# A delta-rule recurrence: the state update from B as two rounds of quarter-row matmuls, and two loads at another place

## The reference, cut to what matters

```python
batch, n_heads, seq, head_dim = (4, 8, 768, 40)

def _attn_ref(r, k, v, w, a, b):
    for t in range(S):
        y[:, :, t] = np.einsum('bhd,bhde->bhe', rt, state)
        Sa = np.einsum('bhde,bhe->bhd', state, at)
        state_decay = state * wt[:, :, None, :] - np.einsum('bhd,bhe->bhde', Sa, bt)
        state = state_decay + np.einsum('bhd,bhe->bhde', vt, kt)

def reference(**kwargs):
    attn_out = _attn_ref(**attn_kwargs)                        # 32 heads, a 40x40 state each
    x = attn_out.transpose(0, 2, 1, 3).reshape(B * S, H * D)   # 3072 tokens of 320
    x = _moe_ref(x=x, **moe_kwargs)     # gate: x @ w_gate + log1p(exp(x @ w_noise)) * noise, the best 2 of 8
    return _moe2_ref(x=x, **moe2_kwargs)                       # dense 320 -> 2048 -> 320
```

## Time and profile before

| what | value |
|---|---|
| median of 3 runs | 1462.92 us (1461.02 to 1466.77) |
| profiled execution | 1462.92 us, span 1461.1 us |
| stage_a, stage_re up to its first expert matmul, the rest | 0 to 541 us, 541 to 588 us, 588 to 1461 us |
| mean granted TensorE clock over the span | 0.926 of full speed |

### The profile page before, as it was taken

How to read it: one execution, slowest core, us unless ns; L and a number is a source line. 1 busy time by engine, 2 the same in 40 slices (tenths; PEclk the granted TensorE clock), 3 DMA queues, 4 the chain that set the end, 5 groups by cost and what they waited for, 6 DMA issues and landing times. The chain is left out here.

```text
span 1461.1 us, 37835 instructions
## 1 busy us (share of the span) xinstructions
PE 1270.4 (87%) x15278; PEld 1159.1 (79%) x15278; DVE 947.4 (65%) x1619; ACT 666.1 (46%) x1453; POOL 304.3 (21%) x262
## 2 busy tenths in 40 slices
PE   4458789778887966999999999999939999999998
PEld 3447577666776755999999999999938888888987
DVE  8978685795938017788788788887825535455343
ACT  3325444444543330567666676776603333333332
POOL 1116262542623221111111111111042012020000
PEclk9998888888988875999999999999969999999999
DMA  6563535536243312877877778778521011010000
GB/s 228 143 161 99 144 119 139 169 111 167 92 113 114 91 25 71 259 239 226 263 229 248 254 210 265 246 226 254 167 77 42 23 33 54 1 54 18 0 19 18
DMA packets 158832, 197.61 MB, mean 135 GB/s; under 512 B 62869, under 2 KB 117373, under 8 KB 158717
## 3 DMA queue, kind: packets, MB, share of 16 engines
q1 hardware_dynamic: 136724, 148.12, 33.5%
q10 hardware_dynamic: 16713, 29.77, 6.5%
q0 software_dynamic: 5280, 18.03, 4.3%
HBM read 171.57 MB, written 24.31 MB: 134 GB/s over the span
## 5 line engine op out<-in xcount | busy, mean ns | idle before, releaser
L350 DVE TENSOR_TENSOR prod<-Tl,Lt 128x1 f32<-128x1 f32 (+30 forms) x186 | 151.9, 817 | 51.4 <-DMA Lt<-lscr 45.3
L1297 DVE TENSOR_TENSOR gf<-psM,low 128x512 f32<-128x512 f32 x96 | 66.3, 691 | 181.1 <-ACT low L1335 169.4
L1335 ACT ACTIVATE low<-psM 128x512 f32<-128x512 f32 x96 | 57.5, 599 | 244.3 <-PE psM L1393 223.5
L1001 PE MATMUL psE<-w2h,hh 128*128 128x320 f32 x496 | 155.7, 314 | 0.0
L1003 PE MATMUL psE<-w2h,hl 128*128 128x320 f32 x496 | 153.3, 309 | 0.0
L1002 PE MATMUL psE<-w2l,hh 128*128 128x320 f32 x496 | 153.2, 309 | 0.0
L1089 POOL DMA_INDIRECT xs<-xrow,src x62 | 60.9, 982 | 410.2 <-PE psE L970 370.8
L986 PE MATMUL psE<-xh,w1h 128*128 128x256 f32 x496 | 141.1, 285 | 1.9 <-DVE xh L833 1.9
L987 PE MATMUL psE<-xl,w1h 128*128 128x256 f32 x496 | 141.0, 284 | 0.0
L988 PE MATMUL psE<-xh,w1l 128*128 128x256 f32 x496 | 140.9, 284 | 0.0
L833 DVE TENSOR_TENSOR w2l<-w2t,w2h 128x320 fp32r<-128x320 f32 x248 | 122.0, 492 | 16.3 <-ACT w2h L828 16.3
(11 more groups left out here) (185 smaller groups left out, 3154.8 us busy)
## 6 DMA issues: line engine op xcount, KB each, us to landing
w2t<-in_w_dram SPq DMA_DIRECT2D x31, 1280.0 KB, 6.8
w1t<-in_w_dram SPq DMA_DIRECT2D x31, 1024.0 KB, 8.9
w1t<-in_w_dram SPq DMA_DIRECT2D x62, 256.0 KB, 9.4
Vd<-in_vG_dram ACTq DMA_DIRECT2D x44, 320.0 KB, 4.8
ysort<-ys SPq DMA_DIRECT2D x31, 320.0 KB, 5.0
RV<-in_rvE_dram ACTq DMA_DIRECT2D x44, 208.0 KB
P<-in_wR_dram SPq DMA_DIRECT2D x24, 209.6 KB
U<-in_wE_dram SPq DMA_DIRECT2D x24, 209.6 KB
```

The lines of the kernel that those rows point to most:

```text
L350: mark(nc.vector.tensor_tensor(prod[:, 0:t, 0:t], Tl[:, 0:t, CH - t:CH], Lt[:, t:t + 1, CH - t:CH].to_broadcast([128, t, t]), ALU.mult))
L1001: mm(o, hh[:, f, sl], w2h[:, f, :], start=(f == 0), stop=False)
```

## The change

Four edits.

1. Pn loses its zeroed copies: it is [128, 4, 2, 40] instead of [128, 4, 2, 2, 40]. ACT still makes two copies a chunk, each of 160 elements a partition instead of 320, with the constant scale -1. half_m is gone. `turn_P` writes its four transposes 104 columns apart instead of 128.
2. `grow_B` contracts over one quarter (32 partitions) at a time, 40 columns, so it has 32 matmul calls a chunk instead of 16. They stand in two rounds: quarters 0 and 2, and then, behind a wait on o_S for the end of the first round, quarters 1 and 3. A call of float32 is two weight loads and two matmuls in the trace.
3. noise and triu are loaded by ACT's queue at the start of `stage_a`, triu in the place of half_m, noise last; nz and triu are allocated for the whole program. The DMAs on SP and the waits on r_nz and r_tu are gone; ACT waits for noise at the end of `stage_a`.
4. The constants array loses its last two columns.

```diff
-        half_m = sb("half_m", [128, 2])
-        Pn = sb("Pn", [128, 4, 2, 2, D])
+        Pn = sb("Pn", [128, 4, 2, D])
@@ ScalarE, start of stage_a
             act.dma_start(ident[:, :], cst[:, 0:128]).then_inc(q["l_c"], 16)
-            act.dma_start(half_m[:, :], cst[:, 480:482]).then_inc(q["l_c"], 16)
+            act.dma_start(triu[:, :], cst[:, 128:256]).then_inc(q["l_c"], 16)
...
             act.dma_start(wx[:, :, :], wgh[:, :, :]).then_inc(q["l_c"], 16)
+            act.dma_start(st["nz"][:, :, :], noise.rearrange("(i p) e -> p i e", p=128)).then_inc(q["l_nz"], 16)
@@ ScalarE, each chunk
-                for z in range(2):
-                    copy(Pn[:, :, :, z, :].rearrange("p g x d -> p (g x) d"), ps[:, 6, :].rearrange("p (g m) -> p g m", m=64)[:, :, 0:D],
-                         "a_Pn" if z else None, scale=half_m[:, z:z + 1])
+                for x in range(2):
+                    copy(Pn[:, :, x, :], ps[:, 6, 0:4 * EP].rearrange("p (g m) -> p g m", g=4)[:, :, 64 * x:64 * x + D],
+                         "a_Pn" if x else None, scale=-1.0)
@@ ScalarE, end of stage_a
+            act.wait_ge(q["l_nz"], 16)
@@ TensorE
-                    m = turn(ps[:, 6, 128 * i:128 * i + EP], PTs[:, i, :], unit)
+                    m = turn(ps[:, 6, EP * i:EP * i + EP], PTs[:, i, :], unit)
-            def grow_B(k):
+            def grow_B(k, f):
                 s, c = slot(k)
                 for b in range(NB):
                     for p in range(2):
-                        for i in range(2):
-                            two = slice(64 * i, 64 * i + 64)
-                            m = mm(ps[E_[p], i, 0:2 * NB * D].rearrange("p (z m) -> p z m", z=2)[:, :, D * b:D * b + D],
-                                   Bk[two, (4 * s + c) % RT, b, p, :], Pn[two, 2 * (b // 2) + p, b % 2, :, :].rearrange("p z d -> p (z d)"),
+                        for h in (f, f + 2):
+                            o = (h % 2) * NB * D + D * b
+                            m = mm(ps[E_[p], h // 2, o:o + D], Bk[Z_[h], (4 * s + c) % RT, b, p, :], Pn[Z_[h], 2 * (b // 2) + p, b % 2, :],
                                    start=False, stop=True, skip_group_check=True)
-                m.then_inc(q["p_S"], 1)
+                m.then_inc(q["p_S" if f else "o_S"], 1)
...
                     pe.wait_ge(q["a_Pn"], k + 1)
-                    pe.wait_ge(q["o_S"], k + 1)
-                    grow_B(k)
+                    pe.wait_ge(q["o_S"], 2 * k + 1)
+                    grow_B(k, 0)
+                if k < NK:
+                    pe.wait_ge(q["o_S"], 2 * k + 2)
+                    grow_B(k, 1)
@@ stage_re: SyncE, TensorE, VectorE
-            sp.dma_start(nz, noise.rearrange("(i p) e -> p i e", p=128)).then_inc(q["r_nz"], 16)
-            sp.dma_start(triu[:, :], cst[:, 128:256]).then_inc(q["r_tu"], 16)
-            pe.wait_ge(q["r_tu"], 16)
-            dve.wait_ge(q["r_nz"], 16)
```

More of the change, by code:

```diff
@@ L43, with stage_a @@
 KE = [(0, 128), (128, 128), (256, 64)]
-def stage_a(nc, st, wE, wR, aE, bE, kE, rvE, vG, cst, wgh, lscr, tscr, xrow):
+def stage_a(nc, st, wE, wR, aE, bE, kE, rvE, vG, cst, wgh, noise, lscr, tscr, xrow):
     ctx = ExitStack()
@@ L55, in stage_a @@
         ps = ctx.enter_context(nc.psum_tensor("psA", [128, 8, 512], F32))
-        LG, ident = st["LG"], st["ident"]
+        LG, ident, triu = st["LG"], st["ident"], st["triu"]
         pos_m = sb("pos_m", [128, CH])
-        half_m = sb("half_m", [128, 2])
         two_m = sb("two_m", [128, 2, CH])
@@ L88, in stage_a @@
         xo = sb("xo", [128, 2, DM])
-        names = ("l_c l_p l_p0 l_p1 l_p2 l_p3 l_u0 l_u1 l_u2 l_a0 l_a1 l_a2 l_b0 l_b1 l_k0 l_k1 l_r0 l_r1 l_r2 l_g0 l_g1 "
+        names = ("l_c l_nz l_p l_p0 l_p1 l_p2 l_p3 l_u0 l_u1 l_u2 l_a0 l_a1 l_a2 l_b0 l_b1 l_k0 l_k1 l_r0 l_r1 l_r2 l_g0 l_g1 "
                  "l_lw l_lane l_tw l_t0 l_t1 l_x0 l_x1 "
@@ L833, in split_lo, with stage_re @@
     return nc.vector.tensor_tensor(lo, src, hi.bitcast(F32), ALU.subtract)
-def stage_re(nc, st, noise, cst, w_in, w_out, w1, w2, xrow, ysort):
+def stage_re(nc, st, w_in, w_out, w1, w2, xrow, ysort):
     ctx = ExitStack()
@@ L905, in stage_re @@
         wr = [sem("e_wr0"), sem("e_wr1")]
[L906 removed]
+        names = ("r_wt r_io r_az r_ex r_dif r_e2 r_M r_PR r_dve r_tx r_lo r_hi r_src r_src0 r_Q "
                  "e_ld2 e_z e_tr e_xh e_xl e_w1h e_w1l e_w2h e_w2l e_mm1 e_hh e_hl e_mm2 e_yA e_yV e_mh e_ml e_mz").split()
@@ L1425, in program @@
         ysort = nc.dram_tensor("ysort", [NTS * TS, DM], F32, kind="Internal").ap()
-        st = {"ident": sb("ident", [128, 128])}
+        st = {"ident": sb("ident", [128, 128]), "triu": sb("triu", [128, 128])}
         xrow = nc.dram_tensor("xrow", [TOK, DM], F32, kind="Internal").ap()
         st["LG"] = sb("LG", [128, NT, 2 * E])
-        stage_a(nc, st, wE, wR, aE, bE, kE, rvE, vG, cst, wgh, lscr, tscr, xrow)
         st["nz"] = sb("nz", [128, NT, E])
-        st["triu"] = sb("triu", [128, 128])
+        stage_a(nc, st, wE, wR, aE, bE, kE, rvE, vG, cst, wgh, noise, lscr, tscr, xrow)
         st["gate"] = sb("gate", [128, 2, NT])
@@ L1438, in program @@
             st[n] = sb(n, [128, F2 // 128, DM], F32R)
-        stage_re(nc, st, noise, cst, w_in, w_out, w1, w2, xrow, ysort)
+        stage_re(nc, st, w_in, w_out, w1, w2, xrow, ysort)
         stage_m(nc, st, ysort, out)
@@ L1474, in layouts @@
     a["wgh"] = g
-    c = np.zeros((128, 482), np.float32)
+    c = np.zeros((128, 480), np.float32)
     c[:, 0:128] = np.eye(128)
```

1 line of the change is left out of this document (removed).

## The result

| | before | changed |
|---|---|---|
| median (least to most) of 5 | 1462.92 us (1460.35 to 1466.77) | 1472.61 us (1465.31 to 1475.69) |
| profiled execution, span | 1462.9, 1461.1 us | 1466.5, 1464.7 us |
| first stage ends | 541.1 us | 547.7 us |
| mean granted clock | 0.926 | 0.928 |

The ratio is 1.0066 [1.0042, 1.0092]: 9.7 us slower, where the forecast was 5.5 us slower. The profiled execution is one of the changed kernel's shortest (+3.6 us), so a cause that doesn't show in every execution must be looked for in more than one profile. In it the first stage is 6.6 us longer, and from its end to the first expert matmul it is 0.8 us less. Behind the first expert matmul the program takes 871.2 us instead of 873.4, where the prediction had no change; the fourteen profiles of this document have 870.8 to 873.4 us there, the kernel before the most.

The account below looks back on a forecast made before the run. No single engine was taken to bound the first stage; the bound passes between PE and DVE. Rounds +6.8, Pn -0.5 and noise -0.8 gave +5.5 on 1462.9, so 1468.4 us, pauses unsized, range 1462 to 1474.

Parts of the forecast that it names:

- The block, +0.62 a chunk: From grow_B's first load to add_K: 0.52 us becomes 1.14 with two rounds, priced from read_S; bounds +0.34 and +0.97.
- The count of 11 chunks: First-stage chunks, 11 of 24, where a longer grow_B costs time because PE is ahead of a wait: +6.8 us.
- The other 13 chunks: First-stage chunks where PE's waits for decay cover the longer grow_B; up to 1.2 us can leak.
- Pn -0.5: ACT's shorter Pn pair, 0.50 us instead of 0.95, ends five PEld waits: -0.5 us, bounds 0 and -1.4.
- noise and triu, -0.8: DVE's DMA wait before the multiply by noise goes: -0.8 us; triu 0; loads at the start 0, with +1 as bound.
- The pauses, the term that was left out of the sum: PE's waits for instructions: 1536 more instructions shift packet borders and move pauses; unsized, nothing by the skill's rule.
- the issue sum before `first` far from 12: Sign of error in the profile after: PE's "issue" waits before first summing far from 12 us.
- The rival with two more pauses on the path: Two more 1.7 us pauses in PE's run gv, first: +3.4, 1471.8 us; chance 0.30.
- The forecast's own range of 4 us: The main forecast's own whole-program range, 1466 to 1470.2 us, given chance 0.35.
- cheap rounds: Rival: grow_B's rounds are cheap or hidden at gv's pace, 0.34 a chunk: +2.4, 1465.3 us; chance 0.23.
- vanishing pauses: Rival: the pauses at 105.40 and 502.96 vanish by the shift: +0.3, 1463.2 us; chance 0.09.
- ACT on the path: Rival: ACT's 0.45 us a chunk is on the path, 10.8 us: 1457.6 us; chance 0.03.

Follow-up runs that it names:

- the rounds alone: Kernel before with the smaller Pn and two rounds of grow_B, noise, triu and half_m unchanged: 1464.06 us, 1.0035; run again 1466.23 us, 1.0048.
- the tiles' places alone: Two rounds of grow_B with nz and triu allocated ahead of the first stage, half_m gone, loads in the second stage as before: 1474.51 us, 1.0097.
- the late loads: Changed kernel with triu and noise issued by ACT in chunk 20 instead of at the program's start: 1476.06 us, 1.0106.
- the second group: Second of three groups of four kernels, each on one chip beside the kernel before (1458.3 us there); the changed kernel measured 1468.78 us, 1.0079.
- four rounds: Changed kernel with grow_B's 32 calls in four rounds of 8 instead of two of 16: 1474.5 us, 1.0113.
- the shifted kernel before: Kernel before with 24 unused 32x32 calls at PE's start, moving every packet border by 96 instructions: 1461.65 us, 1.0011.

## Why the prediction came out as it did

**The block, +0.62 a chunk: right.** 0.57 measured (0.60 and 0.49 instead of 0.59 and 0.55). Its parts were those of `read_S`; the gap at the border of shapes came out near 0.05 instead of 0.15. The rule of the Trainium skill, page "TensorEngine Tiling (Array Packing)", section Key Properties, is borne out in its direction (a border costs something) and is small here.

**The count of 11 chunks: right in sum for the rounds alone, wrong in its shares.** 11 x 0.57 = 6.3 us, less 0.5 for Pn, against 5.1 and 7.9 measured. But superchunk 4 was given two chunks, because before DVE waited for PE only at 437.10. Once PE was later, a wait stood at 455.84 too: a wait of before tells where PE is late, and not where it is nearly late. By that the count there is nearer three or four; it is worth 1.1 us at most, and the 5.0 us that s4 lost hold more than it. Superchunk 2 was given one chunk, and in the profile after DVE doesn't wait for PE there. The other 13 chunks were to be covered by PE's waits for `decay`, which would have shrunk; they stayed at 29.6 us, and it was the waits for `y_out` that gave way. And that one wait for `decay` must be short was true (1.04 us at 239.11) but didn't follow: four times 7.4 is more than 28.4.

**Pn -0.5: right in kind.** The pair takes 0.50 us, and the waits at it are gone.

**noise and triu, -0.8 in the sum: right where it was looked for, and the term that was mis-sized as a whole.** 45.9 instead of 46.7 us stands in the profile of every kernel with the loads moved. But edits 3 and 4 together did not gain. Taking the two measurements of each, the changed kernel (1.0066 and 1.0079) lies 0.31% above the rounds alone (1.0035 and 1.0048), with 0.09 to 0.53 as my interval, or 4.5 us (1.3 to 7.7), where -0.8 was forecast. Every other kernel with the new places of the tiles (1.0070, 1.0072, 1.0097, 1.0106, 1.0111) is above both measurements of the rounds alone, too. The prediction costed these edits at 0 at the start of the program, with +1 as bound, and looked only at the transfers. The kernel with the tiles' places alone, in which no transfer is moved, bears the surcharge, and the late loads don't take it away. What in the places costs it, if it is they, isn't known: the cause stays open.

With it the sum comes out: 6.3 - 0.5 for the rounds and 4.5 for edits 3 and 4 is 10.3 us, against 9.7 (6.1 to 13.5) and, in the second group, 11.5 measured. The forecast of 5.5 lies just below the first interval.

**The pauses, the term that was left out of the sum: found rightly, and not shown to cost anything clear of zero.** The prediction named what would show it ("the issue sum before `first` far from 12"; there it is 9.5, but the sum over all lines went from 14.7 to 29.7), and took zero as the likeliest. All seven pauses before `first` were read as a property of that line. Nearly all of them belong to borders in the instruction stream, and the borders come down wherever the count puts them, in `gv`, `lb` and the Grams too. In each profile of the changed kernel and of the rounds in two the sum was 25 to 30 us, and the kernel before had the lowest of all that were profiled. The count of instructions does not fix the sum, though: four rounds, with the same count, had 17.2 us, and the highest ratio of all. And the cost is much smaller than the sum: 10 us more of pauses in the shifted kernel before came to 1.6 us (-1.0 to 4.1), and the rounds alone, with 12 us more of them than the kernel before, came out at what the block's price gives without any term for pauses. The rival with two more pauses on the path (1471.8) is nearest to the 1472.6, but no run shows its mechanism: it put the pauses in `gv` and `first`, they fell on the Gram matrices as well, and the distance that it happens to fill is that of edits 3 and 4. That is luck.
The page "Runtime: NRT & Kernel Launch" of the Trainium skill, section Instruction fetch mechanics, has the fetch hidden by the pace of issue; the pauses of 2.90, 4.66, 3.53 and 5.66 us shown above, at the borders of its blocks, contradict it. If they cost little here, as it seems, it is not because there are none.

**The clock had no term at all.** The forecast's own range of 4 us was narrower than the 5.4 us that lie between the thirds of the kernel before's executions with the lowest and the highest clock. The profiled execution of the changed kernel, at 0.928, lies 6 us below its median; of the five that the median is taken from, one had 0.932 (1465.3 us) and four 0.922 to 0.926 (1472.1 to 1475.7).

Of the other rivals, cheap rounds are out by the block of 1.09 us, vanishing pauses by their sum, and ACT on the path by ACT's 10 us less of busy time that brought nothing.

Open: through what edits 3 and 4 cost their 4.5 us; whether the pauses cost anything; how much of s4's 5.0 us are pauses, how much the clock; and the count of chunks, which the intervals of the rounds alone leave anywhere between some 6 and 18, with the pauses taken as free.

## What to carry to other kernels

In a stage where no engine sets the pace, a local price times the number of places on the path came within 2 us, when the place was priced from the nearest block of the same shape. What was left over came with edits that the sum took for free: tiles allocated earlier and two loads moved. When a change has several edits, run each alone, and one that "costs nothing" too. Pauses for instructions can move and multiply at any edit of a stream of thousands of short calls; their sum in a profile is no price, since a pause that falls where PE would have waited anyway is covered. Before a forecast of half a per cent, read the granted clock over more than one execution; its scatter alone may be as large.

## What the runs showed of the hardware

- Nearly all pauses of PE without a cause in the profile lie 256 instructions of its stream apart (loads, matmuls and its other instructions counted; at the same remainder in every profile), in runs of equal short calls. Counted where longer than 0.25 us in the first stage, the kernel before had 9 such, the others 13 to 20, and at most 3 elsewhere. Most end 2.2 to 3.1 us after a packet of 16 KB on the instruction queue started, 1.2 to 1.6 us after it ended.
- Splitting a matmul of 64 x 80 columns into two of 40 does not halve it: 64 loads of 64 x 40 took 0.94 us, 32 took 0.58; and a wait of PE on its own round costs 0.20 to 0.23 us whatever the round's size (32 loads or 16).
- With PE busy for 9.5 to 9.8 of each 10 us the granted clock stood at 0.50 to 0.54 for 20 us in one profile, and with PE busy for 8.9 to 9.9 at 0.72 to 1.00 in the same part of the last superchunk in another. Filling a part of the idle gap in front of it put a low clock (0.59) later and didn't prevent it.
